# Sorted mixture of experts: experts in index order with at least one tile each, the first two loaded at the end of the attention

## The reference

```python
for t in range(S):
    y[:, :, t] = einsum(q[:, :, t], state)
    state = state + beta * outer(k_t, v_t - state . k_t)
x = attn_out.transpose(0, 2, 1, 3).reshape(3072, 384)
x = ((x @ w1) * (x @ w2) @ w3) @ w_out
logits = x @ w_gate + modality_bias[modality_id]
e_idx = argmax(logits, 1)
gate_w = softmax(logits)[token, e_idx]
for e in range(8):
    mask = e_idx == e
    if not mask.any():
        continue
    h = relu(x[mask] @ w1[e])
    out[mask] = gate_w[mask, None] * (h @ w2[e])
```

## Time and profile before

| | us |
|---|---|
| median of three runs | 988.99 (986.44 to 989.28) |
| the profiled execution, its own time | 982.71 |
| its span, first to last instruction | 980.8 |
| mean granted TensorE clock | 0.955 of full |

### The profile page before, as it was taken

One profiled execution on the slowest core, in us unless ns is written; L12 is line 12 of the kernel. 1 busy time (PEld: TensorE's weight loads), 2 busy tenths in 40 slices (PEclk: granted clock), 3 DMA queues, 4 the chain that ended last, 5 costly groups with the idle time before them and its releaser, 6 DMA issues.

```text
span 980.8 us, 29550 instructions
## 1 busy us (share of the span) xinstructions
PE 889.7 (91%) x11972; PEld 746.7 (76%) x11973; DVE 497.3 (51%) x891; ACT 343.7 (35%) x628; POOL 277.7 (28%) x296
## 2 busy tenths in 40 slices
PE   4898878999998999899989999997369999999996
PEld 3666556778876887688768878986259898989985
DVE  2456656665675567556755673232356333333332
ACT  1234343443554355435533442221153222222221
POOL 5333333444434443444344421010001101011010
PEclk9999986999999999999989999998579999999998
DMA  7333211111111111111111101100941111111110
GB/s 248 104 103 113 75 37 37 38 38 38 47 39 58 38 44 42 59 38 46 40 59 30 29 23 46 32 34 18 320 181 44 42 42 41 38 41 41 48 42 21
DMA packets 46570, 60.13 MB, mean 61 GB/s; under 512 B 9192, under 2 KB 39160, under 8 KB 45552
## 3 DMA queue, kind: packets, MB, share of 16 engines
q1 hardware_dynamic: 38640, 42.35, 14.4%
q0 software_dynamic: 3200, 9.56, 2.6%
q10 hardware_dynamic: 4608, 6.46, 2.5%
HBM read 42.26 MB, written 11.77 MB: 55 GB/s over the span
## 4 chain that ended last, share of the span: by engine, by line
PE 76%; POOL 7%; DVE 6%; issue 5%; ACT 3%; DMA 1%; SPq 1%; ACTq 0%; POOLq 0%; DVEq 0%
PE banks L1418 17%; PE banks L1543 12%; PE banks L1557 11%; PE banks L1436 10%; PE banks L1278 4%; PE banks L1388 3%; PE banks L1355 2%; PE banks L1574 2%; PE banks L1345 2%; PE banks L1367 2%; PE banks L1238 2%; POOL nm L535 1%; POOL inv L539 1%; DVE corr L873 1%; POOL sorted_rows L555 1%
## 5 line engine op out<-in xcount | busy, mean ns | idle before, releaser
L1418 PE MATMUL banks<-xr,w12r 128*128 128x512 f32 x864 | 226.4, 410 | 0.0
L1418 PEld LDWEIGHTS banks<-xr,w12r 128*128 128x128 f32 x864 | 159.9, 193 | 35.9 <-DVE xr L933 0.2
L1543 PE MATMUL banks<-experts,kept 128*128 x486 | 124.6, 411 | 11.0 <-DVE experts L1170 8.5
L1543 PEld LDWEIGHTS banks<-experts,kept 128*128 128x128 f32 x486 | 92.6, 195 | 32.3 <-issue 11.6
L1557 PE MATMUL banks<-experts,kept 128*128 x624 | 114.8, 340 | 0.0
L1436 PE MATMUL banks<-kept,hr 128*128 128x392 f32 x576 | 112.2, 347 | 0.0
L1557 PEld LDWEIGHTS banks<-experts,kept 128*128 128x128 f32 x624 | 107.1, 188 | 0.0
L1436 PEld LDWEIGHTS banks<-kept,hr 128*128 128x128 f32 x576 | 100.9, 188 | 2.0
L585 POOL DMA_INDIRECT out<-ys,xs x26 | 25.6, 984 | 259.8 <-DVE ys L1205 259.8
L523 POOL TENSOR_TENSOR kb<-keys,beta_sb 128x384 f32<-128x384 f32 x24 | 29.1, 1214 | 245.5 <-PE banks L1377 245.5
L621 ACT ACTIVATE inv<-banks 128x512 f16<-128x512 f32 x96 | 57.2, 596 | 84.9 <-PE banks L1278 72.4
(11 more groups left out here) (144 smaller groups left out, 1338.9 us busy)
## 6 DMA issues: line engine op xcount, KB each, us to landing
raw<-in_moe_w SPq DMA_DIRECT2D x6, 1536.0 KB, 7.3
kq<-in_qT SPq DMA_DIRECT2D x24, 256.0 KB, 2.7
xs<-sorted_rows ACTq DMA_DIRECT2D x28, 197.0 KB, 2.4
kraw<-in_k SPq DMA_DIRECT2D x24, 192.0 KB, 2.3
vals<-in_v SPq DMA_DIRECT2D x48, 96.0 KB, 2.5
w3T<-in_w3T SPq DMA_DIRECT2D x8, 512.0 KB, 4.4
w<-in_w SPq DMA_DIRECT2D x8, 384.0 KB, 4.7
xT<-yT SPq DMA_DIRECT2D x48, 64.0 KB, 2.1
```

The costliest lines, as they stand in the source:

```text
L1418: last = mm(psum[:, UP + w, :], w12r[:, p, w, k, j * P:(j + 1) * P], xr[:, r, k, :], start=(k == 0 and p == r), stop=(k == KT - 1 and p == 1))
L1543: last = mm(psum[:, f, :], xsr[:, w, p, k, :], experts[:, bass.ds(slot * (2 * WE) + at, FF // 2)], start=(k == 0 and p == r), stop=(k == K ...
```

## The change

The experts keep their own numbers and each has at least one tile (`max` with 1), so the table of ranks goes and all eight experts are loaded and split. SP loads the experts 0 and 1 as soon as the attention's buffers are free (`load_expert`), and the other six in order after its four fills. `xs` and `raw` change places in memory. The first expert is split beside the last chunk's down products, at pieces 17, 20 and 21 (`FIRST_SPLITS`; `upper_ahead` on ACT, `lower_ahead` on DVE). Expert 1 is split between the end of the dense block and tile 0: w1 on ACT after the last `exps`, on DVE after the two `take_x`, and w2 on both around the first relu. `table[3, 0]` becomes 1, so that no split stands in tile 0. PE's code is not touched.

```diff
+FIRST_SPLITS = {17: ("w1", 0), 20: ("w1", 1), 21: ("w2", 0)}
...
+        xs = sbuf(late, "xs", [P, TURN, ROW])
         raw = sbuf(late, "raw", [P, SLOTS * WE])
-        xs = sbuf(late, "xs", [P, TURN, ROW])
...
+            def load_expert(k):
+
+                for at, size, name in ((0, KT * FF, "w1"), (KT * FF, FT * DM, "w2")):
+                    since(sp, q[f"expert_{name}_in"], 16 * k)
+                    if k >= SLOTS:
+                        sp.wait_ge(q[f"lower_{name}"], (k - SLOTS + 1) * (2 if name == "w1" else 1))
+                    at_slot = k % SLOTS * WE + at
+                    sp.dma_start(raw[:, at_slot:at_slot + size], a[f"moe2_{name}"][k]
+                                 ).then_inc(q[f"expert_{name}_in"], 16)
+
             sp.dma_start(fill[:], a["fill"]).then_inc(q["b_in"], 16)
             sp.dma_start(numbers[:], a["small"][:, M_STARTS:]).then_inc(q["b_in"], 16)
+            for k in range(SLOTS):
+                load_expert(k)
             sp.wait_ge(q["b_in"], 80)
...
             fill_after(sp, range(0, E, 2))
-            sp.wait_ge(q["ranks_ready"], 1)
-            for k in range(E):
...
-                with sp.If(some > 0):
...
-                        if k == 0 and name == "w2":
-
-                            for w in range(2):
-                                sp.wait_ge(x_in[w], 16)
...
+            for k in range(SLOTS, E):
+                load_expert(k)
...
+                    if c == C - 1 and k in FIRST_SPLITS:
+                        upper_ahead(0, *FIRST_SPLITS[k])
...
+            def upper_ahead(rank, name, f=0):
+                act.wait_ge(q["up_b"], FT * C)
+                if rank:
+                    act.wait_ge(q["down_done"], B * C)
+                act.wait_ge(q[f"expert_{name}_in"], 16 * (rank + 1))
+                src, upper, _ = ahead_of(rank, name, f)
+                nc.scalar.activation(upper, src, ACT.Copy).then_inc(q[f"upper_{name}"], 1)
...
             exps(C - 1)
+            upper_ahead(1, "w1", 0)
+            upper_ahead(1, "w1", 1)
...
-            first = act.value_load(table[0:1, 3, 0:1], min_val=0, max_val=E - 1)
-            split(first, "w1", [0])
             take_x(0, 0)
-            split(first, "w1", [1])
             take_x(1, 1)
+            upper_ahead(1, "w2")
             take_hid(0)
-            split(first, "w2")
...
+            def lower_ahead(rank, name, f=0):
+                dve.wait_ge(q[f"upper_{name}"], 2 * rank + f + 1 if name == "w1" else rank + 1)
+                src, upper, lower = ahead_of(rank, name, f)
+                nc.vector.tensor_tensor(lower, src, upper, ALU.subtract).then_inc(q[f"lower_{name}"], 1)
...
+                    if c == C - 1 and k in FIRST_SPLITS:
+                        lower_ahead(0, *FIRST_SPLITS[k])
...
             link(v.tensor_reduce(ntile[:, 0], over[:], AX.X, ALU.add))
-            link(v.tensor_scalar(ntile[:, 1], ntile[:, 0], 0.0, None, ALU.is_gt))
+            link(v.tensor_scalar(ntile[:, 0], ntile[:, 0], 1.0, None, ALU.max))
...
-            v.memset(table[:, 3, 0:1], 0)
...
+            v.memset(table[:, 3, 0:1], 1)
+            v.tensor_scalar(table[:, 3, 1:], ttab[:, 0], 1.0, float(E - 1), ALU.add, ALU.min
                             ).then_inc(q["table_ready"], 1)
...
             take_x(0, 0)
-            split(first, "w1", [1])
             take_x(1, 1)
+            lower_ahead(1, "w1", 0)
+            lower_ahead(1, "w1", 1)
             take_hid(0)
-            split(first, "w2")
+            lower_ahead(1, "w2")
```

More of the change, by code:

```diff
@@ L216, in program @@
             hot_ready rank_done place_ready row_ready scattered dve_step count_done
-            ranks_ready table_ready fill_ready filled expert_w1_in expert_w2_in upper_w1
+            table_ready fill_ready filled expert_w1_in expert_w2_in upper_w1
             upper_w2 lower_w1 lower_w2 x_done xs_upper x_taken hid_done hid0_ready
@@ L354, in split_expert, with ahead_of @@
                              for ap in places], 2, f)
+        def ahead_of(rank, name, f):
+            at, size = ((f * KT * FF // 2, KT * FF // 2) if name == "w1" else (KT * FF, FT * DM))
+            at_raw, at_hi = rank * WE, rank * 2 * WE
+            if name == "w2":
+                return (raw[:, at_raw + at:at_raw + at + size], experts[:, at_hi + at:at_hi + at + size],
+                        experts[:, at_hi + WE + at:at_hi + WE + at + size])
+            return tuple(t[:, o:o + KT * FF].rearrange("p (k f) -> p k f", k=KT)[:, :, f * FF // 2:(f + 1) * FF // 2]
+                         for t, o in ((raw, at_raw), (experts, at_hi), (experts, at_hi + WE)))
         def next_expert(eng, n):
@@ L465, in _ @@
             fill_after(sp, range(0, E, 2))
-            sp.wait_ge(q["ranks_ready"], 1)
-            for k in range(E):
-                e = sp.value_load(table[0:1, 2, k:k + 1], min_val=0, max_val=E - 1)
-                some = sp.value_load(table[0:1, 2, E + k:E + k + 1], min_val=0, max_val=1)
-                with sp.If(some > 0):
-                    at_slot = k % SLOTS * WE
-                    for at, size, name in ((0, KT * FF, "w1"), (KT * FF, FT * DM, "w2")):
-                        if k == 0 and name == "w2":
-                            for w in range(2):
-                                sp.wait_ge(x_in[w], 16)
[L478 to L486, removed]
+            for k in range(SLOTS, E):
+                load_expert(k)
         @block.gpsimd
@@ L1115, in _, with by_tile @@
             link(v.tensor_reduce(ntile[:, 0], over[:], AX.X, ALU.add))
-            link(v.tensor_scalar(ntile[:, 1], ntile[:, 0], 0.0, None, ALU.is_gt))
-            link(v.tensor_copy(ntile[:, 2:4, 0:1], ntile[:, 0:2, 0:1]))
+            link(v.tensor_scalar(ntile[:, 0], ntile[:, 0], 1.0, None, ALU.max))
+            link(v.tensor_copy(ntile[:, 1, 0:1], ntile[:, 0, 0:1]))
             for e in range(1, E):
-                link(v.tensor_tensor(ntile[:, 2:4, e:e + 1], ntile[:, 2:4, e - 1:e], ntile[:, 0:2, e:e + 1],
-                                     ALU.add))
+                link(v.tensor_tensor(ntile[:, 1, e:e + 1], ntile[:, 1, e - 1:e], ntile[:, 0, e:e + 1], ALU.add))
             tiles = numbers[:, M_TILE - M_STARTS:M_TILE - M_STARTS + TABLE * E].rearrange("p (i e) -> p i e", e=E)
[L1124 to L1137, removed]
+            def by_tile(k):
+                return ntile[:, None, k, :].to_broadcast([P, TABLE, E])
+            v.tensor_copy(table[:, 2, 2 * E:2 * E + 1], ntile[:, 1, E - 1:E])
+            link(v.tensor_tensor(past[:, 0], tiles, by_tile(1), ALU.is_ge))
             link(v.tensor_tensor(past[:, 1], past[:, 0], by_tile(0), ALU.mult))
@@ L1140, in _ @@
             link(v.tensor_reduce(ttab[:, 1], past[:, 1], AX.X, ALU.add))
-            link(v.tensor_tensor(past[:, 1], past[:, 0], by_tile(1), ALU.mult))
-            link(v.tensor_reduce(ttab[:, 2], past[:, 1], AX.X, ALU.add))
             link(v.scalar_tensor_tensor(ttab[:, 1], ttab[:, 1], float(-P),
@@ L1147, in _ @@
             v.tensor_scalar(table[:, 0, 0:TABLE], ttab[:, 1], float(E * CAP), None, ALU.min)
-            link(v.tensor_scalar(ttab[:, 3, 0:1], ntile[:, 3, E - 1:E], -1.0, None, ALU.add))
-            v.tensor_scalar(table[:, 1, 0:TABLE], ttab[:, 2], ttab[:, 3, 0:1], None, ALU.min)
-            v.memset(table[:, 3, 0:1], 0)
-            v.tensor_scalar(ttab[:, 2], ttab[:, 2], 1.0, None, ALU.add)
-            link(v.tensor_copy(ttab[:, 3, 1:2], ttab[:, 3, 0:1]))
-            v.tensor_scalar(table[:, 3, 1:], ttab[:, 2], ttab[:, 3, 1:2], None, ALU.min
+            v.tensor_scalar(table[:, 1, 0:TABLE], ttab[:, 0], float(E - 1), None, ALU.min)
+            v.memset(table[:, 3, 0:1], 1)
+            v.tensor_scalar(table[:, 3, 1:], ttab[:, 0], 1.0, float(E - 1), ALU.add, ALU.min
                             ).then_inc(q["table_ready"], 1)
@@ L1177, in take_x @@
                                 xsr[:, w, 0], ALU.subtract).then_inc(q["x_taken"], 1)
-            first = dve.value_load(table[0:1, 3, 0:1], min_val=0, max_val=E - 1)
-            split(first, "w1", [0])
             take_x(0, 0)
-            split(first, "w1", [1])
             take_x(1, 1)
+            lower_ahead(1, "w1", 0)
+            lower_ahead(1, "w1", 1)
             take_hid(0)
-            split(first, "w2")
+            lower_ahead(1, "w2")
             def tile(i, r):
```

## The result

| | us |
|---|---|
| the changed kernel, median of four runs | 1064.27 (1063.35 to 1065.96) |
| the kernel before, median of four runs | 987.72 (986.05 to 989.28) |
| ratio, with its 95% interval | 1.0777 (1.0750 to 1.0804) |
| profiled execution: its own time, span | 1065.96, 1064.2 |
| mean granted clock | 0.947 |

A forecast was written before the change was run, and what follows sets the result against it. PE alone was taken to bound the kernel from the second tile on. Start -11.6, five added tiles +76.0 and clock +10.0 make +74.4 us, on the median of 988.99 a forecast of 1063.4, range 1049 to 1074.

The forecast's parts named there:

- The count: Tiles and expert loads: five experts without tokens get a tile each, 31 tiles for 26, eight expert loads for three.
- rival B: Tile count: every expert has tokens, so no tile is added and only the start counts, 977.4 us; 3%.
- The chained tile: Five added tiles: each waits for DVE's split of the next expert, period 15.26 us, first 15.0, together 76.0.
- Rival A: Added tiles: they flow at PE's pace of 9.58 us, five cost 47.9, time 1025.3; 5%.
- The clock: PE's rests in the five added tiles: the granted clock falls, 2.0 us each, 10.0 in all, at most 11.8.
- The start: Up to the end of the first down product: earlier load and split gain 11.6 us, bounds 5.3 and 13.4.
- rows that land after 704: Start of the tiles: tile 0's rows expected at 700.5 us; landing after 704 would show the forecast wrong.
- What was costed at nothing: Loads and splits of experts 0 and 1 before the tiles, and weights of experts 2 to 7: all free or hidden.
- rival C: Added tiles: rows or the next expert's w1 land late, 3 us for each of five, time 1078; 9%.
- The base: Whole kernel: forecast set on the median of three runs before, 988.99 us; the profiled execution was 6.3 below it.

The follow-up runs named there:

- The fillers: Changed kernel with eight idle matmuls on PE in the wait of tiles 1, 2 and 3: 1057.53 us, ratio 1.0718 to the kernel before.
- The order experiment: Changed kernel with w1 of the next expert split one tile earlier, ahead of w2, on ACT and DVE: 1032.87 us, ratio 1.0475.
- the tables alone: Kernel before with only the tile counts raised to at least one, its start of the tiles unchanged: 1070.44 us, ratio 1.0858.
- The guard: Changed kernel with SP waiting for the rows of tiles 0 and 1 before it loads expert 2: 1058.49 us, ratio 1.0735.

## Why the prediction was right

*The count.* Five more tiles and ten more half loads, as read from the six transfers and the reference's own counts. This carries the sign and the size; rival B had nothing behind it.

*The chained tile.* Forecast 15.26 and 2.0 for the clock, 17.26; measured 17.33, 17.34, 17.22, 17.16, 17.11. The fillers show the two parts separately, 15.3 to 15.5 and 2.2. The order experiment shows that the order of the splits was the cause, and the releaser of all five waits is DVE's split. The order was changed on ACT and DVE together, and DVE waits 2.5 us a tile for ACT's part of w2, so what each engine's order does alone is not shown. The first of the five, which I had at 15.0 without the clock, took 17.33 with an up product 2.33 over its full pace, so 15.0; from T1 to its up product it is 6.31, as forecast. Rival A (9.58 a tile) is refuted by the trace and by the tables alone at 1070.4.

*The clock.* 10.0 forecast; the five up products are 10.1 us longer than 4.21 each, and it fell in all five rests of 5.4 to 5.7 us. The 2.0 for each was chosen between nothing and 2.35, and single ones were 1.84 to 2.33, so that the sum came out within 0.1 is luck. The sentence quoted from the Trainium skill (TensorE: Matmul & The Clock Gate, What's actually happening) holds for these five alone, as 10.1 of 1064.2 us is 0.95%. It doesn't hold for this kernel as a whole: with the first up product (6.21) it is 12.1 us or 1.1%, and the granted clock is at 0.83 in the mean from 100 to 200 us, too. Leaving this cost out would have missed an eighth of the change's effect.

*The start.* Forecast a gain of 11.6, measured 8.6 by the trace, inside the bounds of 5.3 and 13.4. The step that was mis-sized is the landing of tile 0's rows. I wrote "Expert 2's 3 MB are mostly in by then, so I take 3.5"; it took 6.4, as 3.00 MB were still to come at 700 us. The gain is 3.0 smaller than forecast: 2.9 for this landing and 0.5 for the issue, less 0.35 by which the first up product was shorter (6.21 against 6.56). In the other kernels with this start and no guard the rows landed in 6.4 to 7.4 too. What I had missed is that the weights were themselves held up by the fills and by POOL's indirect writes, so that they met the rows instead of being ahead of them: from 696 to 698 us SP's queue had 23.5% of the engines' time and the other two 84.5%, from 698 to 700 it had all of it. The load was issued 1.2 later than before, against my 0.7 (703.99 against 696.30, less the 6.5 of the dense block). I had named rows that land after 704 as a sign of being wrong. They landed at 710.37, and with the 6.5 taken off at 703.9, just at the edge. The guard shows that the weights beside them are the cause: with it the rows land in 2.4 to 2.5. The 8.6 itself is known to some 1.5 us only: the kernels with the order and with the fillers have the same start, and from the down products to T1 they take 61.1, a gain of 10. The turn-taking of queues named in the Trainium skill (DMA: Bandwidth & Descriptors, Queues, rings and completion order) would have made it 4.8; with one loaded queue beside it, it was 6.4, so by that reading the gain would have been over-estimated too.

*What was costed at nothing.* The loads of experts 0 and 1, the splits beside the down products, and expert 1's w1 ahead of the fills were free: from the end of the last down product to PE's next matmul it is 3.04 us, as it was 3.05. DVE's last split beside the down products ended at 683.9, about 1.2 us before it was needed, where I had half a microsecond. Later weights stayed hidden, with no wait of PE for them, so rival C did not come; in the chain the rows were in time too.

*The base.* The forecast of 1063.4 is 0.9 below the median. That it is so close is luck, as two errors nearly cancel in it: the start gained 3 us less than I said, and the median of before is 1.3 lower with the fourth run. What remains, about 1 us, is less than the scatter of the runs. The profiled execution's own time, forecast as 1057.1, was 1065.96; 6.5 of these 8.9 us are the dense block's later end.

## What to carry to other kernels

When work is padded to a fixed shape so that a lookup can go, cost the padding at the price of the place where it falls, not at the steady price: an empty tile cost 17.2 us here where a full one costs 9.58, since each one brought a preparation that the long run of tiles of an expert hides. In a queue that is the bottleneck for a while, put first what is needed first by the waiting engine: moving w1 ahead of w2 took back 31 of 86 us without taking any work away. And where large early loads are let go, hold them until the small load on the critical path has landed.

## What was not expected of the hardware

A load of 197 KB took 2.4 to 2.5 us with nothing beside it, 6.4 with two weight halves issued before it on another engine's queue, and 8.5 in one case before. It was not an even sharing: from 704 to 708 us the weights' queue had 96.5% of the DMA engines' time and the rows' queue 2.4%. The two halves themselves took 11.6 us beside fills and indirect writes, against 7.3 in the median before. Filling a rest of 5.7 us with idle matmuls kept the granted clock at 2.4 GHz and paid for itself at once, as the time was being waited for anyway.
